# Weighting three batches' tokens inside the last MLP instead of behind it

## The chip, the cores and the metric

One core of a Trainium2 chip runs the whole program. The metric is the device time in microseconds (us), the median of several executions. The engines are TensorE (PE; its weight loads are PEld), VectorE (DVE), ScalarE (ACT), GpSimd (POOL) and SyncE (SP), which issues all the DMAs here. Each engine works through its own list in order and is tied to the others by semaphores.

## What is computed

```python
attn_out = causal attention with decay     # q, k, v: 4 batches x 8 heads x 576 x 64
x = attn_out as (2304 tokens, 512)
h = x @ w_in                               # 512 x 2048
x = (h * sigmoid(1.702 * h)) @ w_out       # 2048 x 512: the MLP

logits = x @ phi                           # 2304 x 32 slots
d = softmax(logits, over all 2304 tokens)  # one weight of every token for every slot
slot_input = d.T @ x                       # 32 x 512: "weighing the tokens"
for e in range(8):                         # 8 experts, 4 slots each
    slot_out[e] = relu(slot_input[e] @ w1[e]) @ w2[e]   # 512 x 1024, 1024 x 512
c = softmax(logits, over the 32 slots)
result = c @ slot_out                      # 2304 x 512
```

The softmax over tokens needs its maximum and its sum over all four batches, so the slot inputs are complete only when the last token of the last batch is known.

## The kernel before, in words

A batch is 576 tokens, `QT` = 5 tiles of up to 128. Attention runs head by head. The MLP of batch m is cut into 64 *units* (`U_MLP`): four quarters of the 2048 hidden columns, and in each 8 up units (kind 0: four tiles of hidden columns for the first 288 tokens, then for the other 288) and 8 down units (kind 1). A unit is 12 matmuls of 288 columns (L1204). Behind an up unit ScalarE takes a tanh (L736) and VectorE writes `hid` (L925); behind a down unit VectorE adds into `x2t` (L930, L932), the MLP's output with the token as column. The results of units alternate between two banks of PSUM (`mb`), so a unit waits for the reading of what was two places before it in the order that `bank_order` writes down (`wait_bank`, L1161). MLP m runs between the attention steps of batch m + 1; the last one, of batch 3, stands alone.

Every engine's order is written out by hand: `batch_steps` and, for the last MLP, `last_units` (L124) give one list of steps that each engine walks, doing its own part of each. In MLP m the steps of batch m - 1 stand between the units (`mlp_steps`, L99): its logits behind unit 0, five `token` steps that transpose `x2t` into `x2tok` (tokens as rows; ScalarE copies them, L722), and `turn` behind unit 6 (`TURN_AT`), two transposes (L1148, L1149) that give the logits with tokens as rows. VectorE then takes maxima and the softmax over slots at the units of `SOFTMAX_AT`.

For the last batch this is done by `post` steps: `("post", 0)` behind unit 61 takes the logits (L1142) and transposes (L1154) of tiles 0 and 1, `("post", 1)` behind unit 63 the rest. Behind it comes the tail: the logits are turned, VectorE takes the maximum of each slot over all batches (L943, L945), spreads it by a matmul (L1221), subtracts it from all 20 tiles of logits (L950), ScalarE exponentiates (L754), TensorE weighs the 20 token tiles in 20 matmuls of 512 columns into four column groups (`dispatch`, L1229), a matmul over `es4` gives the sum (L1238), VectorE scales (`part`, L968), and four matmuls with `sel4` add the groups up (L1243) to `slot_t` (L973). Matmuls on constants (`busy`, L1157) fill waits of TensorE. In fp32 a matmul is two instructions in the trace. Then the eight experts run, `up` (L1256) and down (L1295) each, and last the 20 matmuls of the result (L1312).

The experts' weights are 16 pieces of 2 MB in a ring of ten places: four in `ring_a`, filled by halves at the units with j = 2 of the last MLP, five in `ring_b`, which lie in memory that the MLP uses until its end, and one, `ring_x`, over `x2tok`, filled behind the weighing (SP waits for it). The later ones wait for a place.

## Time and profile before

| | |
|---|---|
| median of 3 runs | 765.5 us (764.19 to 765.57) |
| the profiled execution | 765.94 us, of which span 764.2 us |
| TensorE busy | 717.7 us, 94% |
| VectorE, ScalarE, GpSimd busy | 444.7, 437.0, 399.3 us |
| mean granted TensorE clock | 0.983 of 2.4 GHz |

The span is from the first to the last instruction. The busy shares tell which engine is full; the windows (stretches of time with each engine's busy time) tell where; the chain of waits tells what each step of the end stood behind; the timeline gives single instructions. In the timeline and the groups, brackets at the end of a row give the idle time ahead of an instruction and what ended it. PEclk is the granted clock: 1.00 is 2.4 GHz, 0.50 is 1.2 GHz, and a value between them is a window in which it changed.

### The profile page before, as it was taken

The numbers are of one execution on the slowest core, as the hardware profiler recorded it, in microseconds if no ns is written. First come the engines' busy times: TensorE is split into PE (matmuls) and PEld (weight loads), VectorE is DVE, ScalarE is ACT, GpSimd is POOL, SyncE is SP. The second block draws the span as 40 slices with busy tenths as digits, with TensorE's granted clock in tenths as the row PEclk, the third lists the DMA queues.
The fourth block names the chain that finished last, engine by engine and source line by source line (L and its number), as shares of the span: only waits on it lengthen the run. The fifth ranks groups of instructions, "written<-read, shape, count | busy, mean of one in ns | idle before, by whom it ended". The sixth has DMA issues, their size and how long they took to land.

```text
span 764.2 us, 15776 instructions
## 1 busy us (share of the span) xinstructions
PE 717.7 (94%) x6027; PEld 681.0 (89%) x6027; DVE 444.7 (58%) x1255; ACT 437.0 (57%) x1031; POOL 399.3 (52%) x439
## 2 busy tenths in 40 slices
PE   3999979999999999999999999999999999998993
PEld 3888879999999999999999989999999999995562
DVE  5898957676776646675656466766542332224323
ACT  4788866575757675666576665757554344311113
POOL 4355357474747764565657564848385476520000
PEclk9999989999999999999999999999999999998897
DMA  4433323332333333333331413332214454598976
GB/s 104 106 92 106 94 65 89 87 94 81 95 94 96 95 94 81 87 105 91 100 91 51 126 28 95 94 108 67 69 43 141 135 169 163 161 401 348 357 307 247
DMA packets 90362, 96.65 MB, mean 126 GB/s; under 512 B 61296, under 2 KB 61296, under 8 KB 88240
## 3 DMA queue, kind: packets, MB, share of 16 engines
q1 hardware_dynamic: 90288, 95.66, 40.6%
q8 instruction: 48, 0.79, 0.4%
q14 instruction: 26, 0.21, 0.1%
HBM read 90.84 MB, written 4.79 MB: 125 GB/s over the span
## 4 chain that ended last, share of the span: by engine, by line
PE 79%; DVE 10%; ACT 7%; issue 2%; DMA 0%; POOL 0%; SPq 0%; DVEq 0%; POOLq 0%
PE mb L1204 51%; PE yb L1057 6%; PE zb L1076 6%; PE xb L1103 5%; PE mb L1256 2%; DVE prob L838 2%; PE xb L1037 2%; ACT prob L689 2%; PE yb L1295 1%; ACT xh L713 1%; DVE ptl L844 1%; PE yb L1059 1%; DVE kl L806 1%; DVE qs L802 1%; ACT qs L681 1%
## 5 line engine op out<-in xcount | busy, mean ns | idle before, releaser
L1204 PE MATMUL mb<-xh,wih 128*128 128x288 f32 x512 | 159.1, 311 | 7.8 <-DVE xl L855 4.3
L1204 PE MATMUL mb<-gh,woh 128*128 128x288 f32 x512 | 156.5, 306 | 3.5 <-DVE x2t L932 3.5
L1204 PE MATMUL mb<-xl,wih 128*128 128x288 f32 x512 | 151.6, 296 | 0.0
L1204 PE MATMUL mb<-xh,wil 128*128 128x288 f32 x512 | 151.6, 296 | 0.0
L1204 PE MATMUL mb<-gl,woh 128*128 128x288 f32 x512 | 150.8, 294 | 0.0
L1204 PE MATMUL mb<-gh,wol 128*128 128x288 f32 x512 | 150.8, 294 | 0.0
L643 POOL TENSOR_TENSOR gl<-hid,gh 128x288 fp32r<-128x288 f32 x128 | 105.0, 825 | 74.9 <-ACT gh L730 73.3
L925 DVE SCALAR_TENSOR_TENSOR hid<-gate,mb 128x288 f32<-128x288 f32 x128 | 57.7, 451 | 116.0 <-ACT gate L736 114.9
L689 ACT ACTIVATE prob<-prob,m_row 64x576 f32<-64x576 f32 (+4 forms) x160 | 96.4, 604 | 35.3 <-DVE m_row L824 34.4
L660 POOL TENSOR_TENSOR wol<-stage,woh 128x512 fp32r<-128x512 f32 x64 | 82.9, 1295 | 62.0 <-ACT woh L675 62.0
L660 POOL TENSOR_TENSOR wil<-stage,wih 128x512 fp32r<-128x512 f32 x64 | 82.1, 1290 | 57.0 <-ACT wih L675 56.9
L1204 PEld LDWEIGHTS mb<-xh,wih 128*128 128x128 f32 x512 | 97.2, 190 | 11.4 <-DVE hid L925 5.9
L1204 PEld LDWEIGHTS mb<-gh,woh 128*128 128x128 f32 x512 | 96.3, 188 | 4.4 <-DVE x2t L932 4.4
L736 ACT ACTIVATE gate<-mb 128x288 f32<-128x288 f32 x128 | 52.5, 410 | 80.6 <-PE mb L1204 80.1
L1204 PEld LDWEIGHTS mb<-xl,wih 128*128 128x128 f32 x512 | 97.2, 190 | 0.0
L1204 PEld LDWEIGHTS mb<-xh,wil 128*128 128x128 f32 x512 | 96.9, 189 | 0.0
L1204 PEld LDWEIGHTS mb<-gl,woh 128*128 128x128 f32 x512 | 96.3, 188 | 0.0
L1204 PEld LDWEIGHTS mb<-gh,wol 128*128 128x128 f32 x512 | 96.0, 188 | 0.0
L824 DVE CUSTOM_DVE_ANT_0 prob<-yb,cum_b 64x576 f32<-64x576 f32 (+4 forms) x160 | 83.6, 537 | 11.4 <-issue 10.8
L702 ACT CAST pth<-zb 128x512 fp32r<-128x512 f32 (+1 forms) x128 | 62.7, 490 | 46.3 <-PE zb L1076 45.1
L932 DVE SCALAR_TENSOR_TENSOR x2t<-mb,x2t 128x288 f32<-128x288 f32 x96 | 43.4, 455 | 71.5 <-PE mb L1204 71.3
L844 DVE TENSOR_TENSOR ptl<-zb,pth 128x512 fp32r<-128x512 f32 (+1 forms) x128 | 73.1, 571 | 17.4 <-ACT pth L702 16.6
(196 smaller groups left out, 1471.1 us busy)
## 6 DMA issues: line engine op xcount, KB each, us to landing
stage<-in_moe_w_in SPq DMA_DIRECT2D x64, 256.0 KB, 3.0
stage<-in_moe_w_out SPq DMA_DIRECT2D x64, 256.0 KB, 2.6
ring_a<-in_moe_w SPq DMA_DIRECT2D x16, 1024.0 KB, 6.9
ring_b<-in_moe_w SPq DMA_DIRECT2D x14, 1024.0 KB, 11.8
cum_b<-cum_dram SPq DMA_DIRECT2D x32, 288.0 KB, 3.7
qk_in<-in_q SPq DMA_DIRECT2D x32, 144.0 KB, 3.0
qk_in<-in_k SPq DMA_DIRECT2D x32, 144.0 KB, 3.5
v_in<-in_v SPq DMA_DIRECT2D x32, 128.0 KB, 3.2
```

Of the source, the lines that this page charges most:

```text
L643: pool.tensor_tensor(gl[:, i % FT, HALF * (i // FT):HALF * (i // FT + 1)], hid[:, i % RING, :], gh[:, i % FT, HALF * (i // FT):HALF * (i / ...
L660: pool.tensor_tensor(lo[:, t, :], stage[:, t % 2, :], hi[:, t, :].bitcast(F32), ALU.subtract).then_inc(w_lo, 1)
L689: nc.scalar.activation(prob[0:r, par, POFF[i]:POFF[i] + w], prob[0:r, par, POFF[i]:POFF[i] + w], ACT.Exp, bias=m_row[0:r, par, i:i + 1], s ...
L702: nc.scalar.copy(pth[:, lo:hi], zb[:, c % 2, 0:hi - lo]).then_inc(p_hi, 1)
L736: nc.scalar.activation(gate[:, j % RING, :], bank_of("unit", m, u)[:, 0:HALF], ACT.Tanh, scale=GATE / 2).then_inc(h_tanh, 1)
L824: nc.vector.tensor_tensor_reduce(prob[0:r, par, o:o + w], ybf[0:r, base:base + w], cum_b[0:r, par, 0:w], 1.0, 3e38, ALU.add, ALU.min, m_ro ...
L844: nc.vector.tensor_tensor(ptl[:, lo:hi], zb[:, c % 2, 0:hi - lo], pth[:, lo:hi].bitcast(F32), ALU.subtract).then_inc(p_lo, 1)
L925: nc.vector.scalar_tensor_tensor(out=hid[:, j % RING, :], in0=gate[:, j % RING, :], scalar=1.0, in1=bank[:, 0:HALF], op0=ALU.add, op1=ALU. ...
L932: nc.vector.scalar_tensor_tensor(out=dst, in0=bank[:, 0:HALF], scalar=0.5, in1=dst, op0=ALU.mult, op1=ALU.add).then_inc(unit_out, 1)
L1057: mm(ybf[:, base + k0:base + k0 + kw], qs[:, par, P * i:P * i + P], x[:, par, k0:k0 + kw], start=not last, stop=last, skip_group_check=True)
L1076: ins = tr(zb[:, c % 2, at:at + P], prob[:, par, POFF[i] + P * kt:POFF[i] + P * kt + P], swapped if back else ident)
L1204: ins = mm(bank[:, 0:HALF], a[:, t, P * (j % 4):P * (j % 4) + P], x[:, t, cols], start=(i == 0), stop=(i == 11))
```

## The change

The softmax over tokens of batches 0 to 2 is worked out while the last MLP runs, against the maximum of those three batches: new `early` steps behind units 22 to 34 turn and spread that maximum, exponentiate, weigh 15 token tiles, and keep the result in `acc` and its sum in `all_sum`. The last batch is exponentiated behind the MLP against a maximum that takes in both, still with slots as rows (`et`), turned and weighed in five matmuls; the kept part is multiplied by `kept` and added, and `factor` brings the four column groups to one maximum. `factor` and the reciprocal of the sum go into the selection matrix `sel_f`. The turning of the last batch's logits for the softmax over slots goes behind the slot sums.

`x2tok` is free from then on, so two ring places, `ring_x`, lie over it and are filled from unit 38; the ring has 11 places, and ring pieces loaded during the MLP come in quarters. The post steps are three: `post 1`, between units 62 and 63, transposes the first two of four column blocks of the last tiles. `TURN_AT` goes from 6 to 7, and the filling matmuls from 9, 3, 14 to 2, 3, 3.

```diff
-TURN_AT = 6
+TURN_AT = 7
-BUSY = (9, 3, 14)
+BUSY = (2, 3, 3)
+EARLY = 3 * QT
+EARLY_AT = {"top": 22, "spread": 24, "weigh": 26, "send0": 30, "send1": 31, "send2": 32, "send3": 33, "keep": 34}
+RING_X_AT = 38
...
+        if m == BATCH - 1:
+            steps += [(0, ("early", kind)) for kind in EARLY_AT if EARLY_AT[kind] == u]
     return steps
...
     m = BATCH - 1
-    return (held_steps(m) + mlp_steps(m, 0, U_MLP - 2) + [(0, ("post", 0))]
-            + mlp_steps(m, U_MLP - 2, U_MLP) + [(0, ("post", 1))])
+    return (held_steps(m) + mlp_steps(m, 0, U_MLP - 2) + [(0, ("post", 0))] + mlp_steps(m, U_MLP - 2, U_MLP - 1)
+            + [(0, ("post", 1))] + mlp_steps(m, U_MLP - 1, U_MLP) + [(0, ("post", 2))])
...
-                    if last and j == 2:
+                    if last and u % 2 and u // 8 < len(ring_a):
 
                         sp.wait_ge(x_lo, 4 * BATCH)
-                        load_half_expert(u // 16, u % 16 // 8)
+                        load_expert_part(u // 8, u // 2 % 4, 4)
+                    at = u - RING_X_AT
+                    if last and at >= 0 and at % 2 == 0 and at // 8 < len(ring_x):
+
+                        sp.wait_ge(acc_made, 1)
+                        load_expert_part(len(ring_a) + at // 8, at // 2 % 4, 4)
...
-                elif st == ("post", 1):
+                elif st == ("post", 2):
 
                     sp.wait_ge(unit_done, m * U_MLP + U_MLP - 8)
-                    load_expert(4)
-                    load_expert(5)
+                    load_expert(6)
+                    load_expert(7)
                     sp.wait_ge(w_lo, BATCH * 32)
                     sp.wait_ge(g_lo, BATCH * 32 + RING)
-                    load_expert(6)
+                    load_expert(8)
...
-                elif st[0] == "post":
-                    for i in LAST_POST[st[1]]:
+                elif st == ("early", "weigh"):
+                    act.wait_ge(ew_sub, 1)
+                    nc.scalar.activation(ew[:, :, :], ew[:, :, :], ACT.Exp).then_inc(ew_exp, 1)
+                elif st == ("post", 0):
+                    for i in LAST_POST[0]:
                         act.wait_ge(post_token, m * QT + i + 1)
-                        nc.scalar.copy(x2last[0:QW[i], i, :], last_tokens[i][0:QW[i], :]).then_inc(token_out, 1)
+                        nc.scalar.copy(x2last[:, i, :], last_tokens[i]).then_inc(token_out, 1)
+                elif st == ("post", 1):
+                    for i in LAST_POST[1]:
+                        act.wait_ge(post_token, m * QT + i + 1)
+                        nc.scalar.copy(x2last[0:QW[i], i, 0:P * AHEAD], last_tokens[i][0:QW[i], 0:P * AHEAD]
+                                       ).then_inc(ahead_out, 1)
+                elif st == ("post", 2):
+                    act.wait_ge(max_made, 2)
+                    nc.scalar.activation(et[:, :], last_logits[:, 0:P + 64], ACT.Exp, bias=low_max[:, 1:2],
+                                         accum_out=bsum[:, :]).then_inc(e_made, 1)
+                    nc.scalar.activation(kept[:, :], low_max[:, 0:1], ACT.Exp, scale=-1.0, bias=low_max[:, 1:2]
+                                         ).then_inc(kept_made, 1)
+                    act.wait_ge(post_token, m * QT + QT + 1)
+                    nc.scalar.copy(x2last[:, 2, P * AHEAD:MODEL], last_tokens[2][:, P * AHEAD:MODEL]).then_inc(token_out, 1)
...
+            nc.scalar.activation(factor[:, :], top_back[:, 0:1], ACT.Exp, bias=top[:, 0:1]).then_inc(factor_made, 1)
+            nc.scalar.copy(x2last[:, 3, P * AHEAD:MODEL], last_tokens[3][:, P * AHEAD:MODEL]).then_inc(token_out, 1)
+            nc.scalar.copy(lt[0:SLOTS, P:P + 64], last_logits[0:SLOTS, P:P + 64])
+            nc.scalar.copy(lt[:, 0:P], last_logits[:, 0:P]).then_inc(lt_last, 1)
             act.wait_ge(c_dve, (BATCH - 1) * C_CHAIN + 2)
...
-                elif st == ("post", 1):
+                elif st[0] == "early":
+                    early(st[1])
+                elif st == ("post", 0):
+
+                    nc.vector.memset(last_logits[32:64, P:P + 64], -3e38)
+                    nc.vector.memset(last_logits[64:P, P:P + 64], -3e38).then_inc(edge_made, 1)
+                elif st == ("post", 2):
                     dve.wait_ge(post_logits, m + 2)
-                    keep_turned(last_logits)
-                    dve.wait_ge(lt_turned, m + 1)
-                    keep_logits(last_turn)
-                    keep_maxima(m)
-                    keep_values(m)
+                    nc.vector.tensor_reduce(bmax[:, :], last_logits[:, 0:P + 64], AX_X, ALU.max).then_inc(max_raw, 1)
+                    dve.wait_ge(max_raw, 1)
+                    nc.vector.tensor_scalar(low_max[:, 1:2], bmax[:, :], -1.0, low_max[:, 0:1], ALU.mult, ALU.min
+                                            ).then_inc(max_made, 1)
...
+            def early(kind):
+                if kind == "top":
+                    for i in range(4):
+                        at = ident[32 * i:32 * i + 32, 32 * i:32 * i + 32]
+                        nc.vector.tensor_copy(sel4[32 * i:32 * i + 32, :], at)
+                        ins = nc.vector.tensor_copy(blk4[32 * i:32 * i + 32, :, :],
+                                                    at.unsqueeze(1).broadcast_to([32, 4, SLOTS]))
+                    ins.then_inc(sel_made, 1)
+                    dve.wait_ge(l_kept, 2 * BATCH - 2)
+                    nc.vector.tensor_reduce(gmax[:, :], gm[:, 0:BATCH - 1, :].rearrange("p b s -> p s b"), AX_X, ALU.max
+                                            ).then_inc(gmax_made, 1)
+                elif kind == "spread":
+                    dve.wait_ge(gmax_turned, 1)
+                    nc.vector.tensor_reduce(smax[:, :], top_row[0:SLOTS, 0:P], AX_X, ALU.max).then_inc(smax_made, 1)
+                    dve.wait_ge(smax_made, 1)
+                    nc.vector.tensor_scalar(dmax[:, :], ident[0:SLOTS, 0:SLOTS], smax[:, 0:1], None, ALU.mult
+                                            ).then_inc(dmax_made, 1)
+                elif kind == "weigh":
+                    dve.wait_ge(early_spread, 1)
+                    nc.vector.tensor_tensor(ew[:, :, :], logits[:, :, :],
+                                            top_back[:, 0:SLOTS].unsqueeze(1).broadcast_to([P, EARLY, SLOTS]),
+                                            ALU.subtract).then_inc(ew_sub, 1)
+                    nc.vector.tensor_scalar(low_max[:, 0:1], top_back[:, SLOTS:SLOTS + 1], -1.0, None, ALU.mult
+                                            ).then_inc(max_made, 1)
+                    nc.vector.memset(es4[:, 1:4, :], 0.0)
+                elif kind == "send0":
+                    dve.wait_ge(ew_exp, 1)
+                    nc.vector.tensor_reduce(es4[:, 0, :], ew[:, :, :].rearrange("p t s -> p s t"), AX_X, ALU.add
+                                            ).then_inc(es_made, 1)
+                elif kind == "keep":
+                    dve.wait_ge(early_den, 1)
+                    nc.vector.tensor_copy(all_sum[:, 0:1], top_row[:, 0:1]).then_inc(sum_made, 1)
+                    dve.wait_ge(early_sent, 1)
+                    nc.vector.tensor_copy(acc[:, :], early_sent_ps).then_inc(acc_made, 1)
 
...
-            nc.vector.tensor_copy(slot_t[:, :, :], xb[:, 1, 0:KM * SLOTS].rearrange("p (t s) -> p t s", t=KM)).then_inc(t_dve, 1)
+            m = BATCH - 1
+            dve.wait_ge(max_made, 2)
+            nc.vector.tensor_scalar(top[:, :], low_max[:, 1:2], -1.0, None, ALU.mult).then_inc(top_made, 1)
+            dve.wait_ge(post_token, m * QT + QT + 3)
+            nc.vector.tensor_copy(x2last[0:64, 4, P * AHEAD:MODEL], last_tokens[4][0:64, P * AHEAD:MODEL]).then_inc(token_out, 1)
+            dve.wait_ge(top_turned, 1)
+            nc.vector.tensor_reduce(row_s[:, :], top_row[0:1, 0:P].rearrange("o (g s) -> o s g", g=4), AX_X, ALU.min
+                                    ).then_inc(row_made, 1)
+            dve.wait_ge(row_made, 1)
+            nc.vector.tensor_copy(row[:, :, :], row_s[:, :].unsqueeze(1).broadcast_to([1, 4, SLOTS])).then_inc(row_made, 1)
+            dve.wait_ge(e_turned, 1)
+            nc.vector.tensor_copy(ewt[0:64, 4, :], last_turn[0:64, P:P + SLOTS])
+            nc.vector.tensor_copy(ewt[:, 0:4, :], last_turn[:, 0:P].rearrange("p (i n) -> p i n", n=SLOTS)).then_inc(ewt_made, 1)
+            dve.wait_ge(kept_made, 1)
+            dve.wait_ge(sum_made, 1)
+            nc.vector.tensor_scalar(all_sum[:, 1:2], all_sum[:, 0:1], kept[:, 0:1], bsum[:, 0:1], ALU.mult, ALU.add
+                                    ).then_inc(sum_made, 1)
+            dve.wait_ge(sum_made, 2)
+            dve.wait_ge(factor_made, 1)
+            nc.vector.tensor_tensor(part_sum[:, :], all_sum[:, 1:2], factor[:, :], ALU.mult).then_inc(den_in, 1)
+            dve.wait_ge(den_made, 1)
+            nc.vector.tensor_scalar(den[:, :], top_row[:, 0:1], EPS, None, ALU.add).then_inc(den_added, 1)
+            dve.wait_ge(den_added, 1)
+            nc.vector.reciprocal(rden[:, :], den[:, :]).then_inc(den_added, 1)
+            dve.wait_ge(den_added, 2)
+            nc.vector.tensor_scalar(sel_f[:, :], sel4[:, :], factor[:, 0:1], rden[:, 0:1], ALU.mult, ALU.mult
+                                    ).then_inc(sel_scaled, 1)
+            dve.wait_ge(sent, 1)
+            dve.wait_ge(acc_made, 1)
+            nc.vector.scalar_tensor_tensor(out=acc[:, :], in0=acc[:, :], scalar=kept[:, 0:1], in1=last_sent,
+                                           op0=ALU.mult, op1=ALU.add).then_inc(acc_made, 1)
+            dve.wait_ge(slots_summed, 1)
+            nc.vector.tensor_copy(slot_t[:, :, :], slot_ps[:, 0:KM * SLOTS].rearrange("p (t s) -> p t s", t=KM)).then_inc(slot_made, 1)
+            dve.wait_ge(lt_last_turned, 1)
+            keep_logits(last_turn_l)
+            dve.wait_ge(logits_out, 1 + 2 * m + 2)
+            token_max(m)
+            token_sub(m)
...
+                    pe.wait_ge(unit_out, m * U_MLP + U_MLP + 2 - 4)
+                    pe.wait_ge(edge_made, 1)
                     pe.wait_ge(logits_out, 1 + 2 * m)
+                    pe.wait_ge(acc_made, 1)
                     pe.wait_ge(token_out, 1 + m * QT)
-                    slot_logits(last_logits, LAST_POST[st[1]]).then_inc(post_logits, 1)
-                    for i in LAST_POST[st[1]][0:2]:
-                        turn_last(i)
+                    slot_logits(last_logits, LAST_POST[0], 0, KM).then_inc(post_logits, 1)
+                    for i in LAST_POST[0]:
+                        turn_last(i, 0, KM).then_inc(post_token, 1)
+                elif st == ("post", 1):
+                    pe.wait_ge(unit_out, m * U_MLP + U_MLP + 2 - 2)
+                    for i in LAST_POST[1]:
+                        turn_last(i, 0, AHEAD).then_inc(post_token, 1)
+                elif st == ("post", 2):
+                    pe.wait_ge(unit_out, m * U_MLP + U_MLP + 2 - 1)
+                    slot_logits(last_logits, LAST_POST[1], 0, KM - 1)
+                    pe.wait_ge(unit_out, m * U_MLP + U_MLP + 2)
+                    slot_logits(last_logits, LAST_POST[1], KM - 1, KM).then_inc(post_logits, 1)
+                    pe.wait_ge(ahead_out, len(LAST_POST[1]))
+                    for i in LAST_POST[1]:
+                        turn_last(i, AHEAD, KM).then_inc(post_token, 1)
...
+            def early(kind):
+                if kind == "top":
+                    pe.wait_ge(gmax_made, 1)
+                    pe.wait_ge(logits_out, 1 + 2 * (BATCH - 1))
+                    pe.wait_ge(token_out, 1 + (BATCH - 1) * QT)
+                    tr(top_row[0:SLOTS, 0:P], gmax[:, :], ident[:, :]).then_inc(gmax_turned, 1)
+                elif kind == "spread":
+                    pe.wait_ge(dmax_made, 1)
+                    pe.wait_ge(sel_made, 1)
+                    mm(top_back[:, 0:SLOTS], ones[0:SLOTS, :], dmax[:, :], start=True, stop=True)
+                    mm(top_back[:, SLOTS:SLOTS + 1], blk4[0:SLOTS, :, :].rearrange("p g s -> p (g s)"), smax[:, :],
+                       start=True, stop=True).then_inc(early_spread, 1)
+                elif kind == "keep":
+                    pe.wait_ge(es_made, 1)
+                    mm(top_row[:, 0:1], es4[:, :, :].rearrange("p r s -> p (r s)"), ones[:, 0:1], start=True, stop=True
+                       ).then_inc(early_den, 1)
+                elif kind != "weigh":
+                    pe.wait_ge(ew_exp, 1)
+                    first = 4 * int(kind[-1])
+                    for t in range(first, min(first + 4, EARLY)):
+                        g = t % 4
+                        ins = mm(early_sent_ps[32 * g:32 * g + SLOTS, :], ew[:, t, :], x2tok[:, t, :],
+                                 start=(t < 4), stop=(t + 4 >= EARLY), skip_group_check=True)
+                    if first + 4 >= EARLY:
+                        ins.then_inc(early_sent, 1)
+
+            def slot_logits(bank, tiles, t0, t1):
+
+                for t in range(t0, t1):
                     for i in tiles:
...
+                    if kind == "turn":
+                        pe.wait_ge(token_out, 1 + QT * m + QT)
...
+            tr(top_row[0:1, 0:P], low_max[:, 1:2], ident[:, :]).then_inc(top_turned, 1)
+            busy(BUSY[0], last_sent)
+            pe.wait_ge(e_made, 1)
+            turn_slots(last_turn, et).then_inc(e_turned, 1)
+            pe.wait_ge(row_made, 2)
+            mm(top_back[:, 0:1], row[:, :, :].rearrange("o g s -> o (g s)"), ident[0:1, 0:1], start=True, stop=True
+               ).then_inc(top_spread, 1)
+            busy(BUSY[1], last_sent)
+            pe.wait_ge(ewt_made, 1)
+            pe.wait_ge(token_out, 1 + QT * BATCH)
+            for i in range(QT):
+                g, r = i % 4, QW[i]
+                ins = mm(last_sent[32 * g:32 * g + SLOTS, :], ewt[0:r, i, :], x2last[0:r, i, :],
+                         start=(i < 4), stop=(i > 0), skip_group_check=True)
+            ins.then_inc(sent, 1)
+            pe.wait_ge(den_in, 1)
+            mm(top_row[:, 0:1], blk4[:, :, :].rearrange("p g s -> p (g s)"), part_sum[:, :], start=True, stop=True
+               ).then_inc(den_made, 1)
+            pe.wait_ge(lt_last, 1)
+            turn_slots(last_turn_l, lt).then_inc(lt_last_turned, 1)
+            busy(BUSY[2], top_back)
+            pe.wait_ge(sel_scaled, 1)
+            pe.wait_ge(acc_made, 2)
             for t in range(KM):
-                ins = mm(xb[:, 1, SLOTS * t:SLOTS * t + SLOTS], part[:, :].rearrange("p (n t) -> p t n", t=KM)[:, t, :], sel4[:, :],
-                         start=True, stop=True, skip_group_check=True)
-            ins.then_inc(t_pe, 1)
-            pe.wait_ge(t_dve, 10)
+                ins = mm(slot_ps[:, SLOTS * t:SLOTS * t + SLOTS], acc[:, :].rearrange("p (n t) -> p t n", t=KM)[:, t, :],
+                         sel_f[:, :], start=True, stop=True, skip_group_check=True)
+            ins.then_inc(slots_summed, 1)
```

## Rows read from the trace of the kernel before

**Rows 1.** The page, part 1: busy us, share of the span, instructions.

```profile
PE 717.7 (94%) x6027; PEld 681.0 (89%) x6027; DVE 444.7 (58%) x1255; ACT 437.0 (57%) x1031; POOL 399.3 (52%) x439
```

**Rows 2.** Windows, last MLP: length, then PE, PEld, DVE, ACT, POOL busy; PEclk, DMA, GB/s.

```profile
660.00:680.00 20.00, 20.00 (x153) 20.00 (x152) 5.65 (x13) 8.13 (x20) 11.30 (x12) 1.00 0.72 266
```

**Rows 3.** Windows of 2 us in the tail and the experts.

```profile
700.00:702.00 2.00, 1.84 (x8) 1.84 (x8) 0.73 (x3) 0.00 (x0) 0.00 (x0) 0.76 0.77 295
...
710.00:712.00 2.00, 2.00 (x52) 1.22 (x47) 0.00 (x0) 0.38 (x1) 0.00 (x0) 0.68 1.00 422
...
740.00:742.00 2.00, 2.00 (x66) 1.63 (x66) 0.22 (x1) 0.38 (x1) 0.00 (x0) 1.00 0.10 39
...
748.00:750.00 2.00, 1.88 (x6) 1.49 (x7) 1.10 (x3) 1.15 (x2) 0.00 (x0) 0.71 0.00 0
...
752.00:754.00 2.00, 2.00 (x10) 1.65 (x9) 1.84 (x4) 1.83 (x5) 0.00 (x0) 0.94 1.02 353
```

**Rows 4.** Windows of 1 us, and the timeline's row, at an earlier pause of TensorE.

```profile
100.00:101.00 1.00, 0.00 (x0) 0.00 (x0) 1.00 (x1) 1.00 (x2) 0.82 (x1) 0.66 0.00 0
...
107.00:108.00 1.00, 1.00 (x9) 1.00 (x8) 0.00 (x0) 0.00 (x0) 0.92 (x3) 0.93 0.00 0
...
101.49 0.61 PE L1204 MATMUL mb<-xh,wih 128*128 128x288 f32 x1 [4.29 <-DVE xl L855]
```

**Rows 5.** The chain that ended last: start us, us, what.

```profile
686.62 0.47 DVE x2t L932
...
694.11 4.50 PE xb L1232 x40
...
700.16 2.09 PE xb L1243 x8
...
702.62 3.64 PE mb L1256 x32
...
707.42 3.53 PE mb L1256 x32
...
713.86 1.84 PE mb L1256 x32
...
743.10 1.97 PE yb L1295 x64
```

**Rows 6.** Timeline at batch 0's turn in MLP 1; batch 1's, 161 us later, is alike.

```profile
288.19 0.33 PE L1148 MATMUL mb<-ident,lt 128*128 128x128 f32 x1 [0.78 <-ACT x2tok L722]
...
288.99 0.40 PE L1204 MATMUL mb<-xh,wih 128*128 128x288 f32 x1 [0.36 <-DVE hid L925]
```

**Rows 7.** Timeline, an up unit of the last MLP on ScalarE and VectorE.

```profile
609.88 0.41 ACT L736 ACTIVATE gate<-mb 128x288 f32<-128x288 f32 x1 [4.15 <-PE mb L1204]
...
610.32 0.45 DVE L925 SCALAR_TENSOR_TENSOR hid<-gate,mb 128x288 f32<-128x288 f32 x1 [1.56 <-ACT gate L736]
```

**Rows 8.** Timeline behind unit 61, where `post 0` stands.

```profile
681.31 1.07 PE L1142 MATMUL yb<-x2t,phi_sb 128*32 128x128 f32 x16
...
681.41 0.46 DVE L932 SCALAR_TENSOR_TENSOR x2t<-mb,x2t 128x288 f32<-128x288 f32 x1 [1.14 <-PE mb L1204]
...
682.30 1.09 PE L1154 MATMUL zb<-ident,x2t 128*128 128x128 f32 x8
```

**Rows 9.** Timeline, small steps of the tail.

```profile
690.52 0.37 DVE L943 TENSOR_REDUCE gmax<-gm 128x32 f32<-128x128 f32 x1
...
691.26 0.28 DVE L945 TENSOR_REDUCE smax<-zb 32x1 f32<-32x128 f32 x1 [0.38 <-PE zb L1217]
...
691.88 0.40 PE L1221 MATMUL zb<-dmax,ones 32*128 32x32 f32 x2
...
693.21 0.72 DVE L955 COPY sel<-ident 32x32 f32<-32x32 f32 x4
...
694.57 0.13 PEld L1232 LDWEIGHTS xb<-x2tok,ew 128*32 128x32 f32 x4 [0.30 <-issue]
...
698.54 0.38 PE L1238 MATMUL zb<-ones,es 128*128 128x1 f32 x2
```

## What I expect, and why

> **What bounds the kernel now.** I read the page's busy shares first, then windows along the span, then the chain of waits of the last 95 us, then single rows. TensorE is busy 94% of the span [rows 1], and in the last MLP it has no idle time at all while the other engines have plenty [rows 2]. So in that stretch every instruction, and every wait, that TensorE gets in addition moves the end by its full length. The second limit is the tail behind the last MLP unit: in the chain, the last write of `x2t` starts at 686.62 and the first expert's `up` at 702.62 [rows 5]. That is 16.0 us in which one small step waits for another, 4.50 us of it the 20 matmuls that weigh tokens and 2.09 us the four that sum the slots. Behind it the experts run on TensorE: an `up` takes 1.84 us at the full clock, but the first two take 3.64 and 3.53 [rows 5], because the granted clock is at its lower level for 10.2 us (shares below 1.00 in the windows 700 to 712, all of them 0.50 between those two) [rows 3]. The expert loads are no limit: the DMA share drops to 0.10 at 740 [rows 3] and the last `down` starts at 743.10 [rows 5].
>
> So the question is what moves into a stretch where TensorE has no slack, and what that takes out of the tail.
>
> **What the change adds to the last MLP.** All engines walk the same list, and each early step stands behind the unit of its number. N is the moment at which TensorE would have gone on. The last unit result is read 0.10 us after N (681.31 against 681.41) and an `x2t` result is written by N+0.56 [rows 8].
> 1. Step `top` (behind unit 22): TensorE's transpose waits for `gmax`, but VectorE comes to its part only when it has written unit 22's `hid`: tanh from N+0.10, then 0.44 us to `hid`, then 0.45 [rows 7], so N+0.99. Then come eight copies: four of 32x32, which took 0.72 in a row [rows 9], and four of 32x128, which no row shows; between 0.4 (half of the small ones) and 1.1 (three quarters of a 128x128 reduce, each), I take 0.85. Then `gmax`, 0.37 [rows 9]. TensorE waits 2.95 us and transposes for 0.13: 3.1 us.
> 2. Step `spread` (behind unit 24, a down unit): `x2t` until N+0.56, then from `smax` to the matmul 0.62 [rows 9]: a wait of 1.2 us. Then two pairs of small matmuls at about 0.33 each (0.38 for the like pair [rows 9]): 1.85 us.
> 3. `send0` to `send3`: 15 of the 20 weighing matmuls. They run four at a time: 20 in 4.50 us [rows 5], 0.90 a round; 15 are four rounds, 3.6 us.
> 4. `keep`: 0.35 us [rows 9]. What VectorE and ScalarE do for `weigh` and `keep` lies beside units on engines that are idle most of the time [rows 2], so it costs nothing; without that cover it would be some 3 us.
> 5. `post 0` now waits for two small memsets that stand behind unit 61's `x2t` (N+0.56) [rows 8]. No row shows a memset of 64 columns in PSUM; between 0.1 and 0.4 for both, I take 0.25: 0.8 us. Before, this step waited for nothing.
> 6. `post 1`: six transposes between units 62 and 63; eight took 1.09 [rows 8], so 0.75.
>
> Together 10.4 us, bounds 9.2 to 11.7. Queued behind these waits on TensorE are the next units, and everything later waits for them.
>
> The loads change too: ring pieces go in quarters, one at each odd unit, and two more pieces from unit 38. Each is an issue in SyncE's queue ahead of weight loads, and the queue now waits for `acc` at unit 38, made three units earlier. TensorE never waited for weights in this MLP [rows 2], so I price it at nothing (at worst 1 us); two of twelve late pieces leave the tail's loads, which were not the limit anyway.
>
> **The turn one unit later.** In MLPs 1 and 2 TensorE stands 0.78 us at the turn for ScalarE's copy of token 4 and then 0.36 us before unit 7 for the previous unit's `hid` [rows 6]. Unit 7 will stand in the turn's place and inherit the first wait (same bank rotation); the second goes, since attention work lies before unit 8. Twice 0.36, some given back: -0.5 us (0 to -0.7). In the last MLP the turn waits for nothing.
>
> **What leaves the tail.** From the last `x2t` (0): the logits run mostly ahead of it and end at 1.05; maximum of 192 columns and its comparison 0.55, so 1.6. Exponential (below the 0.41 of a 288-column tanh [rows 7], plus reading its sum) 2.2. Meanwhile transposes, two row steps on VectorE, one matmul, the factor and then ScalarE's last token copy end at about 3.95; this, not the exponential, releases the five weighing matmuls. They are two rounds (the fifth shares its column group with the first): 1.8, so 5.75. Denominator matmul 0.4 [rows 9], three short VectorE steps 0.6, folding `acc` 0.8: about 7.4. Slot sums 2.1 [rows 5], copy 0.35: 9.85. Against 16.0 the tail is 6.1 us shorter (bounds 5.0 and 7.3: the ScalarE copy off the path is 0.5 more; the fifth matmul beside the others 0.7).
>
> That fifth matmul is where a page bears on the sum. By proportion to the 20 in 4.50 us, five would take 1.1 us. The Trainium skill (TensorE: Matmul & The Clock Gate, Part 3: Packing small matmuls) has matmuls in different column groups overlap almost wholly, so that a pack costs about one matmul; by that rule five in four groups cost two packs, 1.8 us. The trace agrees: their weight loads come four together and then pause 0.30 us [rows 9].
>
> **The clock.** TensorE gets two new pauses, 2.95 and 1.2 us, in the MLP. Here the row nearest is the 4.29 us pause at 97 to 101 us: the clock went to 1.2 GHz during it and stayed there for 6.8 us (0.68 of the window 100 to 101, 0.14 of 107 to 108, six between) [rows 4]. The tail fell too [rows 3], behind a pause of 1.24 us among light matmuls (from 698.92 [rows 9] to 700.16 [rows 5]); the shortest low stretch is 3.4 us, around 748 to 754 (0.71, 0.50, 0.94 in two-microsecond windows, the first and the last in [rows 3]). A pause of 2.95 is nearer to the first kind, so I take a fall, of the shortest length: work at half pace for 3.4 us costs 1.7 us (0 to 3.9, when the `spread` pause prolongs it). In the tail I expect the same fall as before and the same slow first two `up`s: the new chain is no denser in TensorE work.
>
> **Sum.** 10.4 - 0.5 - 6.1 + 1.7 = +5.5 us. The profiled execution took 765.94 us with a span of 764.2, the median is 765.5; the difference goes on the median: **771.0 us**.
>
> **Rivals.**
> - The MLP pauses don't lower the clock: 1.7 less, 769.3. For it: no row shows a fall for a pause under 4 us amid dense work. Against: the tail's fall.
> - The fall is prolonged by the second pause two units later, as 6.8 and 10.2 us lows do occur: 3.9 instead of 1.7, 773.2.
> - Other side: the clock stays at 2.4 GHz throughout, since the shorter tail has less light work before the first `up`. It is worth 1.80 + 1.69 us on the two `up`s, 0.4 on the slot sums, 0.4 around them, about 4.3: 769.3 - 4.3 = 765.0. With the additions at their lower bound, 9.2, it is 763.8; faster by 0.2% from additions below 9.4. Against it: the new tail still has some 4 us with hardly any matmul before `up`.
> - Something unpriced in the tail or the stalls moves it by more than my bounds, either way.
>
> **How the numbers follow.** Forecast 0.50 (own range 769 to 773), first rival 0.20, second 0.13, third 0.12, rest 0.05. The range 766.5 to 774.5 leaves out the third rival and the outermost ends. A measurement can tell about 0.2% (1.5 us) from no change. Faster 0.08 (half the third rival, a little of the rest); same 0.11 (its other half, the low end of the first); slower 0.81.
>
> **What would show it.** Right: in the changed kernel TensorE idles about 3 us behind unit 22 for VectorE's `gmax` and 1.2 us behind unit 24 for `dmax`; the last `x2t` comes some 10 to 12 us later than 686.62; from it to the first `up` it is about 10 us; a window near unit 23 has a clock below 1.00. Wrong: no such idle rows, a tail under 8.5 us, or first `up`s of 1.84 us. The forecast fails most easily if the clock holds in both places.

## The result, and the profile after

| | before | changed |
|---|---|---|
| median, measured beside each other | 765.5 us (764.19 to 766.06, 4 runs) | 774.4 us (773.41 to 777.63, 4 runs) |
| the profiled execution | 765.94 us, span 764.2 | 777.63 us, span 775.8 |
| start of the last MLP unit's `x2t` | 686.62 | 704.87 |
| from there to the first `up` | 16.00 us | 10.08 us |
| from the first `up` to the end of the span | 61.6 us | 60.9 us |

The medians differ by 8.8 us, where the forecast was 5.5. The ratio that goes with the interval is 1.0126 (95% interval 1.0092 to 1.0160); it follows the means of the same runs, which differ by 9.6 us. The last MLP became longer than forecast; the tail became as much shorter as forecast. The profiled execution lies at the long end of its kernel's runs, so its rows are read here beside those of a second profile of the same kernel (the first experiment).

The page, part 1 (busy us, share, instructions), to be read against [rows 1]. TensorE is busy 4.6 us longer and has a smaller share, so it also idles 7 us more (53.5 us of the span against 46.5). Whether the busy time is more work or the same work at a lower clock, the windows below tell.

```profile
PE 722.3 (93%) x6018; PEld 684.1 (88%) x6018; DVE 446.4 (58%) x1268; ACT 437.3 (56%) x1039; POOL 399.5 (51%) x439
```

The waits of TensorE between 600 and 765 us of the changed kernel: who waited, for what, us in total, times, longest. Before, [rows 2] showed a last MLP with none; now it has three, and the first two are 1.5 and 0.9 us longer than the 2.95 and 1.2 of the forecast.

```profile
PE zb L1294 <- DVE gmax L979: 4.4, 1, 4.4
PE zb L1298 <- DVE dmax L985: 2.1, 1, 2.1
...
PE yb L1320 <- DVE x2t L1064: 1.0, 1, 1.0
```

Windows of the same profile (columns as in [rows 2]). The clock falls in the first pause and works at its lower level (1.2 GHz) until 629.5, goes up just ahead of the second pause, and is down again from 633 to 636.7. In the tail it is down around the first `up` only; [rows 3] had it down for both.

```profile
622.00:623.00 1.00, 0.00 (x0) 0.00 (x0) 0.97 (x5) 0.00 (x0) 0.43 (x1) 0.84 0.72 145
...
626.00:627.00 1.00, 1.00 (x6) 1.00 (x6) 0.00 (x0) 0.10 (x1) 0.00 (x0) 0.50 0.00 0
...
629.00:630.00 1.00, 0.70 (x4) 0.39 (x2) 0.27 (x1) 0.30 (x1) 1.00 (x2) 0.75 0.00 0
...
633.00:634.00 1.00, 1.00 (x6) 1.00 (x6) 0.00 (x0) 0.00 (x0) 0.00 (x0) 0.50 0.87 350
...
636.00:637.00 1.00, 1.00 (x8) 1.00 (x7) 0.00 (x0) 0.00 (x0) 0.00 (x0) 0.83 0.99 406
...
716.00:718.00 2.00, 2.00 (x24) 0.60 (x16) 0.00 (x0) 0.27 (x1) 0.00 (x0) 0.50 0.35 131
```

**A ledger of the last MLP.** I took the start of VectorE's step of each unit (`hid` or `x2t`) in both traces and subtracted. The difference grows only where the change has put something:

| behind unit | what | growth, us | forecast |
|---|---|---|---|
| 0 | offset at the start | -0.4 | -0.5 |
| 20 to 26 | `top`, `spread`, the clock | 11.8 | 6.65 |
| 30 to 33 | the four sends | 4.8 | 3.6 |
| 34 | `keep` | 0.2 | 0.35 |
| 61 | `post 0` | 1.0 | 0.8 |
| 62 | `post 1` | 0.7 | 0.75 |
| 63 | all of it | +18.25 | +11.6 |

(Another 0.2 us came between units 0 and 20.) The 11.8 split as follows: the work of `top` and `spread` is 0.83, which a trace without pauses and without a fall shows by itself (the combination below); the pauses are 4.45 + 2.10; what is left, 4.4, is the low clock.

**Why the pauses are longer.** The timeline of the changed kernel (rows as in [rows 7]) from unit 20 on. TensorE has finished unit 22 at 619.1 and waits until 623.59.

```profile
618.82 0.62 ACT L746 CAST woh<-stage 128x512 fp32r<-128x512 f32 x1 [2.11 <-DMA stage<-in_moe_w_out]
...
620.16 0.81 DVE L1044 TENSOR_TENSOR cw<-e,r 128x160 f32<-128x160 f32 x1
...
620.74 1.69 POOL L714 TENSOR_TENSOR gl<-hid,gh 128x288 fp32r<-128x288 f32 x2
620.89 0.44 DVE L1057 SCALAR_TENSOR_TENSOR hid<-gate,mb 128x288 f32<-128x288 f32 x1
...
621.25 0.39 DVE L974 COPY sel<-ident 32x32 f32<-32x32 f32 x1
...
621.79 0.67 DVE L974 COPY sel<-ident 32x32 f32<-32x32 f32 x1
...
622.61 0.17 DVE L974 COPY sel<-ident 32x32 f32<-32x32 f32 x1
...
623.59 0.39 PE L1294 MATMUL zb<-ident,gmax 128*32 128x128 f32 x1 [4.45 <-DVE gmax L979]
```

Three things are to be seen. First, ScalarE stood 2.11 us for a weight load, and the tanh of units 21 and 22 stand behind that cast in its queue; so `hid` of 22 is written at 621.33, not 0.99 us after 619.14. Second, part of that delay is VectorE's own: unit 22's tanh is done at 620.38, but VectorE is still in `cw` (620.16 to 620.97), the last step of the softmax over slots of batch 2, so `hid` starts 0.5 us later. `cw` takes 0.81 us here and 0.33 in the tail of the same trace, where GpSimd is idle. Third, the same copy of 32x32 takes 0.17, 0.39 or 0.67 us: the 0.67 one ends at 622.46, just as GpSimd's pair of subtractions does (620.74 + 1.69 = 622.43). The second pause shows the latter alone:

```profile
629.22 2.49 POOL L731 TENSOR_TENSOR wil<-stage,wih 128x512 fp32r<-128x512 f32 x2
...
630.41 1.33 DVE L985 TENSOR_SCALAR dmax<-ident,smax 32x32 f32<-32x32 f32 x1
...
631.80 0.40 PE L1298 MATMUL zb<-dmax,ones 32*128 32x32 f32 x2 [2.10 <-DVE dmax L985]
```

`dmax` took 228 ns in the tail of before, where GpSimd is idle; here 1.33 us, and it ends at 631.74, GpSimd at 631.71.

### The profile page after: what moved, and what is told of

The parts are those of the page before. It is cut to its first block, busy times and chain, and to the rows that moved or that the text cites. A ratio compares the mean times of both kernels' runs of the same rounds, so it can differ in the third digit from the quotient of the medians.

```text
span 775.8 us, 15796 instructions
## 1 busy us (share of the span) xinstructions
PE 722.3 (93%) x6018; PEld 684.1 (88%) x6018; DVE 446.4 (58%) x1268; ACT 437.3 (56%) x1039; POOL 399.5 (51%) x439
## 4 chain that ended last, share of the span: by engine, by line
PE 78%; DVE 10%; ACT 7%; issue 2%; DMA 1%; POOL 1%; SPq 0%; DVEq 0%; ACTq 0%; POOLq 0%
PE mb L1384 50%; PE yb L1194 6%; PE zb L1213 5%; PE xb L1240 5%; PE mb L1434 2%; PE xb L1174 2%; DVE prob L930 2%; ACT prob L760 1%; DVE ptl L936 1%; ACT xh L784 1%; PE yb L1473 1%; PE yb L1196 1%; DVE kl L898 1%; DVE qs L894 1%; DVE xst L942 1%
## 5 line engine op out<-in xcount | busy, mean ns | idle before, releaser
L1384 PE MATMUL mb<-gh,woh 128*128 128x288 f32 x512 | 158.3, 309 | 3.5 <-DVE x2t L1064 3.5
```

What stands on the lines that cost most here:

```text
L1384: ins = mm(bank[:, 0:HALF], a[:, t, P * (j % 4):P * (j % 4) + P], x[:, t, cols], start=(i == 0), stop=(i == 11))
```

## The experiments

My theory after reading the two traces: (a) the ring quarters make a weight load late, (b) VectorE's 32x32 copies and `dmax`, which read and write SBUF, are held up by GpSimd, (c) the resulting pause lowers TensorE's clock, which costs several us more, and (d) the sends cost more than their matmuls. The rivals: the longer pauses are all of one cause, and the clock doesn't matter.

### 1. The changed kernel again

No edit.

> The changed kernel again, on the chip of the other runs of this group, so that each can be compared with it. 774 us, 1.012 of the kernel before. Its trace should show the waits of TensorE behind units 22 and 24 again (4.4 and 2.1 us) and low granted clock once or twice in the last MLP; if the clock is what makes its runs differ by 4 us, the share of low clock differs with the time.

Measured: 774.67 us against 763.85, ratio 1.0139 (1.0106 to 1.0172). Its span is 771.6, 4.2 less than in the first profile. The waits tell most of why.

```profile
PE zb L1294 <- DVE gmax L979: 4.1, 1, 4.1
PE zb L1298 <- DVE dmax L985: 1.0, 1, 1.0
```

`top` again waits over 4 us, but `dmax` was made between two GpSimd steps and the second pause is half as long; the clock falls once (621.4 to 628.1). Units 20 to 26 grow by 8.8: 0.8 of work, 5.1 of pauses, 2.9 of clock. So 4.4 and 2.9 us are the two prices of the low clock in these two traces, and 3.0 of the 4.2 us between them arise in these units, nearly all from the second pause and the second fall. Another 0.9 lies ahead of the last MLP, and 0.4 behind the first `up`. Two traces don't show that this is what makes the runs differ in general: the mean granted clock is 0.980 in both, because this execution has a fall near the start of the program, which the first hasn't.

### 2. TensorE's parts two units behind VectorE's

```diff
-EARLY_AT = {"top": 22, "spread": 24, "weigh": 26, ...
+EARLY_AT = {"top": 20, "top_pe": 22, "spread": 23, "spread_pe": 25, "weigh": 26, ...
```

VectorE makes `gmax` behind unit 20 and `dmax` behind 23; TensorE's parts stand behind 22 and 25.

> VectorE's parts of the first two early steps stand two units ahead of TensorE's (behind units 20 and 23, TensorE's behind 22 and 25); all work is the same. Theory (the pauses of TensorE in the MLP and the low clock behind them are the loss): both waits go (6.5 us in the changed kernel's trace), no low clock in the last MLP (some 4 us), so 10 us less than the changed kernel, 763.5 to 765.5, at or a little below the kernel before. Rival (the added matmuls, the smaller gaps and the tail are the loss): at most 2 us less than the changed kernel, 772.

Measured: 769.50 us, ratio 1.0063 (1.0043 to 1.0083). One pause of 1.2 us is left, no window of the last MLP has a clock below 1.00, and units 20 to 26 grow by 2.5 instead of 8.8 to 11.8. So 5 us of the loss are two waits and the clock that they lower; they are no work. What is left of the pause is cause (b) at its clearest, in the timeline of this kernel:

```profile
619.20 1.27 POOL L731 TENSOR_TENSOR wol<-stage,woh 128x512 fp32r<-128x512 f32 x1 [0.41 <-ACT woh L746]
619.29 1.22 DVE L974 COPY sel<-ident 32x32 f32<-32x32 f32 x1
```

A copy that takes 0.17 us takes 1.22 and ends at 620.51, 0.04 us behind GpSimd's subtraction.

The time fell short of what I expected, 763.5 to 765.5, and did better than the rival's 772. I had taken off the waits and the low clock of the first profile (6.5 and some 4 us), in which both were larger than in the second, and had kept nothing for the pause that is left.

### 3. The pause filled

```diff
 if kind == "top":
-    pe.wait_ge(gmax_made, 1)
     pe.wait_ge(logits_out, 1 + 2 * (BATCH - 1))
     pe.wait_ge(token_out, 1 + (BATCH - 1) * QT)
+    busy(24, top_back)
+    pe.wait_ge(gmax_made, 1)
```

> 24 constant matmuls (3.1 us) stand in TensorE's first pause, behind unit 22, into a free bank; the pause keeps its length. Theory (the idle time lowers the clock): the granted clock stays 1.00 behind unit 22, the wait that is left is under 1.5 us, and the kernel gains the 3 to 4 us that the low clock costs: 770 to 771. Rival (the low clock has another cause, or costs nothing because the engine waits for others then): 774, as the changed kernel, with low clock behind unit 22 as before.

```profile
618.78 2.79 PE L1338 MATMUL zb<-ident_r 128*128 128x128 f32 x24
...
623.13 0.28 PE L1295 MATMUL zb<-ident,gmax 128*32 128x128 f32 x1 [1.56 <-DVE gmax L979]
```

TensorE stands as long as before (2.8 us of filling, 1.6 idle), but the clock holds, and units 20 to 26 grow by 6.3: 2.5 less than in the second profile of the changed kernel, whose pauses are nearly the same (4.1 and 1.0 us), and 5.5 less than in the first, of which about 1.1 is the shorter second pause and the rest the two falls. In this one trace filling the pause kept the clock up. The median is 774.33 us, ratio 1.0135 (1.0091 to 1.0179): no gain against 774.67, and the 770 to 771 that I expected missed. In its profile the clock is low in the tail for 10 us (707.6 to 717.7), both first `up`s take 3.6 us, and from the first `up` to the end it is 63.8 us against 60.5 and 60.9 in the two profiles of the changed kernel. That is the longest such stretch of all the traces (59.4 to 61.6 us in the other twelve). Whether the gain is given back there each time, or this execution's tail was a poor one, stays open.

### 4. The ring loads by halves again

```diff
-if last and u % 2 and u // 8 < len(ring_a):
+if last and j == 2:
     sp.wait_ge(x_lo, 4 * BATCH)
-    load_expert_part(u // 8, u // 2 % 4, 4)
+    load_expert_part(u // 16, u % 16 // 8, 2)
```

> The four ring_a pieces are loaded as before the change, in halves at the units with j = 2, instead of quarters at each odd unit; ring_x as in the changed kernel. Theory (a quarter put ahead of a weight load makes it late, ScalarE stands 2.1 us at the cast of that load and its tanh is late, which lengthens TensorE's first pause from some 3.1 to 4.4 us): the pause is 3.0 to 3.3 us, the kernel gains 1 to 1.5 us, 773. Rival (the late load is chance, or the halves do the same): pause 4.4 us, no gain.

The DMA issues of 614 to 620 us in the changed kernel, then those of 611 to 615 us in this one (issues, KB each, median us to landing): a weight load of 256 KB takes 4.7 us with quarters right ahead of it and behind it (the load is issued at 614.12, one quarter at 612.32, two from 614.49 on), and 2.6 us with a half behind it.

```profile
ring_a<-in_moe_w SPq DMA_DIRECT2D x2, 512.0 KB, 6.0
stage<-in_moe_w_out SPq DMA_DIRECT2D x1, 256.0 KB, 4.7
```

```profile
stage<-in_moe_w_out SPq DMA_DIRECT2D x2, 256.0 KB, 2.6
```

ScalarE's cast then waits for nothing, and the pause at `top` is 2.95 us instead of 4.1 to 4.6:

```profile
622.89 0.29 PE L1294 MATMUL zb<-ident,gmax 128*32 128x128 f32 x1 [2.95 <-DVE gmax L979]
...
629.75 0.53 PE L1298 MATMUL zb<-dmax,ones 32*128 32x32 f32 x2 [1.86 <-DVE dmax L985]
```

So (a) is 1.2 to 1.5 us of the first pause. The time: 774.02 us, ratio 1.0125 (1.0088 to 1.0161), the same as the changed kernel within the measurement; the gain of 1 to 1.5 us that I expected is not seen in it. The clock still fell behind the shorter pause, `dmax` was held again, and the clock fell a second time behind it: 4.9 us of low clock in this trace.

The size of the piece is not what makes a load late. With halves another weight load, issued at 618.10, 2.8 us behind the half of 615.29, took 4.7 us; nothing waited for it. And in the changed kernel the load of 611.95, with a quarter issued right behind it, took 2.5. Late were the loads that had a ring transfer shortly ahead of them; the quarters put one ahead of the load that matters.

### 5 and 6. The turn alone

```diff
-TURN_AT = 6
+TURN_AT = 7
```

in the kernel before, and nothing else.

> The kernel before with the turn one unit later and nothing else. Theory (of the two waits at each turn of MLPs 1 and 2 the one of 0.36 us goes, the one of 0.78 us is inherited by unit 7): the rows of the last MLP come 0.3 to 0.7 us earlier than in the kernel before against the same execution's middle of batch 1, total 763 to 765, not to be told from the kernel before. Rival: the turn's place brings a new wait at unit 8 and nothing is gained.

> The kernel before with the turn one unit later and nothing else, now timed in five rounds. My theory: at each of the two turns one of the two waits goes (0.36 us), so the median is 0.5 us shorter, ratio 0.9993, within 0.2% of 1. Rival: the 2.6 us by which the single execution of this kernel lay below the median was real, ratio 0.997; then something else than the two waits moved. Other rival: the later softmax of the batch costs elsewhere, ratio above 1.001.

One execution took 762.39 us. Timed again it is 762.83 us (12 runs) against 764.18 (18 runs), ratio 0.9985 (0.9973 to 0.9997): 1.1 us faster, with an interval from 0.2 to 2.1. The waits of TensorE from 280 to 292 us, of before and then of this kernel:

```profile
PE mb L1148 <- ACT x2tok L722: 0.8, 1, 0.8
PE mb L1204 <- DVE hid L925: 0.7, 2, 0.4
```

```profile
PE mb L1204 <- ACT x2tok L722: 0.8, 1, 0.8
PE mb L1204 <- DVE hid L925: 0.3, 1, 0.3
```

The unit inherits the first wait of [rows 6] and the second is gone, as forecast. That makes 0.7 us for the two turns; the 1.1 lies above it by less than the interval. This is the fastest kernel measured in this case.

### 7. The sends in one block

```diff
-"send0": 30, "send1": 31, "send2": 32, "send3": 33, "keep": 34
+"send0": 30, "send1": 30, "send2": 30, "send3": 30, "keep": 32
```

> The 15 weighing matmuls of the changed kernel stand all behind unit 30 instead of four behind each of units 30 to 33. They added 4.77 us there, 1.19 for each four against 0.90 in a row. Theory (0.25 to 0.3 us are lost at each change between them and the units' matmuls): they add 3.8 to 4.0 us in one block, 0.8 less in all. Rival (the four matmuls themselves are slower in the MLP, by loads or reads of the ring's transfers): 4.7 us again.

Timelines of the changed kernel, then of this one:

```profile
643.60 1.06 PE L1310 MATMUL xb<-x2tok,ew 128*32 128x512 f32 x8
```

```profile
640.15 3.63 PE L1310 MATMUL xb<-x2tok,ew 128*32 128x512 f32 x30
```

Four by four the sends move the units by 1.19 us each, 4.77 in all; in one block by 3.76, near the 3.6 forecast. So a round costs 0.9 as in the tail of before [rows 5], and the three further changes from units to sends and back cost 1.0 together, 0.34 each. (The kernel: 773.07 us in one execution.)

### 8. The lock by itself

```diff
+if last and 36 <= u < 60:
+    nc.vector.tensor_scalar(probe_s[:, u - 36, :], ident[0:SLOTS, 0:SLOTS], smax[:, 0:1], None, ALU.mult)
+    nc.vector.tensor_scalar(probe_p[:, u - 36, :], top_row[0:SLOTS, 0:SLOTS], 1.0, None, ALU.mult)
```

> The changed kernel with two extra VectorE instructions behind each of units 36 to 59: the 32x32 tensor_scalar of dmax (SBUF to SBUF) again into a scratch, and one of the same size that reads PSUM. Theory (the SBUF one waits while GpSimd has an instruction running, which made dmax take 1.33 us once and 0.23 us in the kernel before): its duration is 0.2 us where GpSimd is idle and up to 1.3 us where a GpSimd instruction is running, and it ends when that ends; the PSUM one stays near 0.2 us throughout. Rival (the semaphore wait or the small size made it slow): both have one duration wherever GpSimd is. The time of the kernel says little, 772 to 778.

The changed kernel with the `dmax` step repeated behind 24 units, from SBUF, and a twin that reads PSUM. The timeline of three units:

```profile
666.25 0.22 DVE L1069 TENSOR_SCALAR probe_s<-ident,smax 32x32 f32<-32x32 f32 x1
666.39 0.17 DVE L1070 TENSOR_SCALAR probe_p<-zb 32x32 f32<-32x32 f32 x1
666.99 1.30 POOL L733 TENSOR_TENSOR wil<-stage,wih 128x512 fp32r<-128x512 f32 x1 [2.56 <-ACT wih L748]
...
667.85 0.48 DVE L1069 TENSOR_SCALAR probe_s<-ident,smax 32x32 f32<-32x32 f32 x1
668.25 0.17 DVE L1070 TENSOR_SCALAR probe_p<-zb 32x32 f32<-32x32 f32 x1
668.84 1.30 POOL L733 TENSOR_TENSOR wil<-stage,wih 128x512 fp32r<-128x512 f32 x1 [0.54 <-ACT wih L748]
...
669.45 0.72 DVE L1069 TENSOR_SCALAR probe_s<-ident,smax 32x32 f32<-32x32 f32 x1
```

With GpSimd idle the step takes 0.22 us; issued while GpSimd runs it takes what is left of GpSimd's instruction (668.33 against 668.29; 670.17 against 670.14). The longest of the 24 took 1.38 us. The twin from PSUM takes 0.17 each time, but it always stands behind the other, mostly when GpSimd is done, so it says less. The Trainium skill (SBUF — State Buffer, section "SBUF: two separate sides") calls the port pair of VectorE and GpSimd an exclusive lock that the first one holds for its whole instruction, on VectorE's side only for steps in a two-port mode or with two SBUF inputs; these rows agree with it.

Not every VectorE step on SBUF is held. `gmax`, a maximum over `gm` in SBUF, takes 0.26 us with GpSimd idle, and as much in the middle of a GpSimd instruction. In experiment 11 the first of this pair of subtractions runs until 621.3:

```profile
620.51 1.64 POOL L714 TENSOR_TENSOR gl<-hid,gh 128x288 fp32r<-128x288 f32 x2
...
621.02 0.25 DVE L980 TENSOR_REDUCE gmax<-gm 128x32 f32<-128x96 f32 x1
```

(The probe kernel: 774.87 us in one execution.)

### 9. The combination

Experiment 2 with `top` behind unit 19 and its copies in a step of their own behind 14, the sends in one block, `keep` behind 32, the two memsets of `post 0` in `keep`, the ring by halves.

```diff
-EARLY_AT = {"top": 22, "spread": 24, "weigh": 26, "send0": 30, "send1": 31, "send2": 32, "send3": 33, "keep": 34}
+EARLY_AT = {"set": 14, "top": 19, "top_pe": 22, "spread": 23, "spread_pe": 25, "weigh": 26, "send0": 30, "send1": 30, "send2": 30, "send3": 30, "keep": 32}
```

> All of it together: VectorE's part of the first step behind unit 19 and of the second behind 23, TensorE's behind 22 and 25, the eight copies behind unit 14, the 15 matmuls in one block behind unit 30, the two memsets of the edge at unit 32, ring_a in halves. Theory: of the 9.7 us by which the last unit was late with the first of these alone, 1.3 (wait behind unit 22), 0.9 (block), 1.0 (edge) go; the last unit is some 6 to 6.5 us late, the tail 6 shorter, so 763.5 to 766.5, no different from the kernel before, 0.997 to 1.003. Rival (the tail's or the experts' lower clock decides more than that): 768 to 770.

Measured: 766.21 us (12 runs) against 765.03, ratio 1.0023 (1.0006 to 1.0039). One window over nearly the whole last MLP of this kernel shows TensorE without a pause and with the full clock:

```profile
600.00:690.00 90.00, 90.00 (x691) 86.62 (x691) 30.34 (x79) 32.22 (x74) 46.68 (x46) 1.00 0.68 238
```

The last unit is 5.46 us late: `top` and `spread` 0.83, the sends 3.76, `keep` 0.22, `post 1` 0.67, `post 0` nothing. That is the pure work moved; the tail gives back 5.9. With all that was found avoidable avoided, the change still brings no gain: the median is 1.2 us above that of before, and the interval of the ratio lies wholly above 1 (0.5 to 3.0 us). By this sum it should have come out 0.4 us ahead. The mean granted clock over its 12 runs is 0.983, over the 17 runs of before beside them 0.986, so some low clock comes on top in many of its executions; where it lies isn't known.

### 10. Its tail filled

```diff
-BUSY = (2, 3, 3)
+BUSY = (2, 3, 8)
...
 ins.then_inc(slots_summed, 1)
+busy(3, top_back)
 pe.wait_ge(slot_made, 1)
```

> The combination (ratio 1.0023, last unit 5.5 us late, tail 5.9 us shorter), with five more constant matmuls of 128 columns in the 0.74 us pause ahead of the slot sums and three in the 0.38 us pause behind them. Theory: TensorE's clock falls at 699.5 because of the pauses just ahead; with them filled it holds through the first up, which then takes 1.84 instead of 3.64 us and the slot sums lose some 0.3 of their length: 1.5 to 2.1 us less, ratio 0.9995 to 1.0005. Rival: the fall comes from the light work since 692 (small matmuls of few rows and columns), not from two short pauses; then it falls at the same place, the first up takes 3.6 us, and the fill costs up to 0.4 us of late start: ratio 1.0023 to 1.003.

Measured: 766.62 us, ratio 1.0035 (1.0020 to 1.0051). The pauses are filled, and the clock falls all the same:

```profile
700.40 2.05 PE L1417 MATMUL xb<-sel_f,acc 128*128 128x32 f32 x8 [0.18 <-DVE acc L1101]
702.26 0.88 PE L1336 MATMUL zb<-ident_r 128*128 128x128 f32 x3
703.07 3.60 PE L1434 MATMUL mb<-ring_a,slot_t 128*4 128x256 f32 x32
```

Three constant matmuls that took 0.55 us at the full clock take 0.88 here. So these two pauses are not what lowers the clock in the tail; my theory for this run fell. That it is the light work since the last unit fits, but was not tried by itself.

### 11. The copies alone moved

```diff
-EARLY_AT = {"top": 22,
+EARLY_AT = {"set": 14, "top": 22,
```

> The changed kernel with the eight copies of VectorE's part of top moved to a step of their own behind unit 14. Theory of two causes: the pause at top was 4.4 us in the changed kernel, of which 1.3 is the late weight load (which stays here) and the rest VectorE's own part; without the copies (some 1.9 us with the time they stood behind GpSimd) it is 2.2 to 2.8 us. The copies behind unit 14 stand beside units and delay TensorE by nothing. Rival: only the late load matters, the copies were hidden behind it: the pause stays 3.5 us or more. Whether the clock falls at a pause of 2.2 to 2.8 us is open: none of that length has been seen in the last MLP without a fill, 1.6 did not and 3.0 did.

```profile
618.59 0.62 ACT L746 CAST woh<-stage 128x512 fp32r<-128x512 f32 x1 [1.79 <-DMA stage<-in_moe_w_out]
...
621.32 0.28 PE L1295 MATMUL zb<-ident,gmax 128*32 128x128 f32 x1 [2.10 <-DVE gmax L980]
```

The late load is still there, and the pause is 2.1 us (2.2 to 2.8 were expected) instead of 4.1 to 4.6: the copies were 2.0 to 2.5 of it. With the 1.2 to 1.5 of experiment 4, both causes are shown. The clock fell behind this pause of 2.1 us too, for a shorter stretch (0.74 of the window 622 to 623, 0.56 of 625 to 626). TensorE had been at work again for 1.2 us when it fell. Units 20 to 26 grow by 5.8, of which 3.2 are pauses, 0.8 work and 1.8 the clock. One execution took 772.38 us.

**Does a pause of this length always lower the clock?** All kernels of this case have the same pause near 20 us, in the first attention steps, where TensorE waits for `kl`. The rows of the kernel before and of the second profile of the changed kernel:

```profile
19.95 0.58 PE L1057 MATMUL yb<-kh,qs 128*128 128x288 f32 x1 [3.24 <-POOL kl L617]
```

```profile
20.59 0.53 PE L1194 MATMUL yb<-kh,qs 128*128 128x288 f32 x1 [3.24 <-POOL kl L688]
```

In the first the clock stays at 1.00 in every window around it; in the second it falls (0.82 in the window 20 to 21, 0.50 from 21 to 24). Over the 13 traces it held in nine and fell in four (experiments 1, 7 and 8 and the second trace of the turn, where the pause was 3.24 to 3.51 us). So the length alone doesn't decide. That in the last MLP every unfilled pause of 2.1 us and more at `top` was followed by a fall is six traces of six, and no rule.

## Why the prediction failed, step by step

The direction, the place of the loss and the tail were right. Of the signs that I named, the two idle rows, the low clock near unit 23 and a tail of about 10 us are there; the last `x2t` came 18.3 and 14.4 us late in the two profiles, not 10 to 12. What failed is the size of the additions: the profiled execution has 18.5 us where the forecast, low clock included, had 12.1.

- **The ring quarters ("I price it at nothing")** is the step that failed by its reason. I argued that TensorE never waited for weights in [rows 2], and asked only what a late load does to TensorE. The load was late for ScalarE, whose queue holds the tanh behind the cast, in front of a step on which TensorE waits without any slack. It cost 1.2 to 1.5 us, experiment 4.
- **`top`, 2.95 us.** It was 4.1 to 4.6 in the four traces with this step in full. Without the late load it is 2.95, the forecast to the digit, but by errors that cancel: the copies took 1.8 us for 1.57, 0.5 of it behind GpSimd, and `gmax` 0.26 for 0.37. A bound from the same small copies in a stretch where GpSimd is idle [rows 9] was no bound: of an instruction's length it left out who else runs.
- **`spread`, 1.2 us** measured 1.0 to 1.2 in five traces and 1.9 and 2.1 in two, by whether GpSimd was at work when `dmax` came. Its row was taken from the tail too [rows 9]. The matmuls of both steps came to 0.83 against 0.78.
- **The clock, 1.7 us.** The fall was forecast with the right place, but its price was the shortest low stretch of the trace. It measured 2.6 to 2.9 where it fell once and 4.4 and 4.9 where the second pause renewed it (and 1.8 behind the 2.1 us pause of experiment 11). That renewal was my second rival; its mechanism is in two of the five traces, and it is not needed for the median: with one fall and the short second pause the sum is 0.8 + 4.4 + 1.1 + 2.8 + 4.8 + 0.2 + 1.0 + 0.7 = 15.8 us in the MLP, less 5.9 in the tail and 0.5 at the turn, 9.4; 8.8 was measured. The likeliest value and the row it came from disagreed: I had said that a pause of 2.95 is nearest to [rows 4], whose low stretch was 6.8 us, and then took 3.4.
- **The sends, 3.6 us** were 4.8. The matmuls were costed right (3.76 in a block); what it costs to go from units to sends and back was not counted.
- **`keep`, `post 0`, `post 1`:** 0.22, 1.04 and 0.66 against 0.35, 0.8 and 0.75. The two memsets, bounded by 0.1 and 0.4, take 0.29 from the first to the end of the second.
- **The turn, -0.5 us:** right in the waits (0.7 in the trace); alone it measured -1.1 (-0.2 to -2.1). That the ledger's first row shows -0.4 is luck: over the 12 traces with the turn moved, unit 0 of the last MLP comes 1.4 us earlier to 0.4 us later than in the trace of before.
- **The tail, -6.1 us:** -5.9. (The terms up to the folding of `acc` add up to 7.55 where the prediction wrote 7.4; 7.53 was measured.) The chain of waits of the changed kernel goes the way that was worked out: it is ScalarE's last token copy that releases the five weighing matmuls, these take two rounds' time, and `acc`, not the denominator, is last ahead of the slot sums.

```profile
708.26 0.27 ACT x2last L843
...
708.66 2.04 PE mb L1406 x10
...
711.66 0.75 DVE acc L1102
...
712.54 2.04 PE xb L1418 x8
...
714.95 3.57 PE mb L1434 x32
```

The rule on packs of the Trainium skill (TensorE: Matmul & The Clock Gate, Part 3: Packing small matmuls) held: 2.04 us, not 1.1. Against [rows 5] one of the two slow `up`s is gone in this profile and in the second; in experiment 3 both were there. That is no effect of the change: with only the turn moved, the kernel before has one slow `up` too, in both its traces. Over all 13 traces the first `up` is always slow (3.14 to 3.64 us), the second fully slow (3.53) in two. This phase of the clock differs between executions.

The range ended at 774.5; 1.0126 of 765.5 is 775.1. It was too narrow because the copies and `dmax` were bounded by rows of the tail, where GpSimd is idle, the late load by a guess of 1 us, and the clock by 3.9, where 4.4 and 4.9 occurred.

## What to carry to other kernels

When small steps are moved from a quiet stretch into a dense one, their durations don't move with them: price VectorE's SBUF copies and products with GpSimd at work, and each queue that feeds a wait, not only the engine that bounds. Put the engine with no slack two or three units behind the step it needs; here that was worth 5 of the 9 us. Keeping the copies out of the way, the sends in one block and the memsets early gave some 3 more. What is left is pure work, 5.5 us, for which the freed 5.9 us of the tail were no more than an even exchange.

## What the runs showed of the hardware

- A 32x32 copy or product of VectorE from SBUF to SBUF takes 0.16 to 0.23 us with GpSimd idle. Issued while GpSimd is in an instruction of 0.8 to 1.3 us it takes up to 1.38 us and ends within 0.05 us of that instruction. In two rows, `dmax` of the first profile among them, it was issued in the last 0.1 us of one GpSimd instruction and held until the end of the next. A maximum from SBUF (128x96, 0.26 us) was not held.
- Among dense matmuls of the last MLP, the clock fell in or behind unfilled pauses of TensorE of 2.1 us (once) and of 2.95 to 4.6 us (five traces of five). Where the longest idle stretch was 1.2 or 1.6 us, in one trace each, it held. Early in the program it held through a pause of 3.24 us in nine traces of thirteen.
- A weight load of 256 KB landed after 4.7 us with a ring transfer issued 1.8 us (512 KB) or 2.8 us (1 MB) ahead of it in SyncE's queue; with one issued behind it only, after 2.5 and 2.6.
- Alternating the column-packed matmuls with the units' ordinary ones cost 0.34 us for each further return trip.
